# A fused attention and mixing kernel: the last two outputs of a step's second half are written to the tiles of the folds

## The reference, cut to what matters

```
# 1. attention, 8 heads of 64: a pooled softmax attention (tokens averaged in fours), repeated back,
#    plus a banded one (|i - j| < 4)                          -> x  [4, 576, 512]
# 2. mixing:
X = fft(fft(x, axis=1), axis=2);  u = x + real(X)
un = (u - mean(u)) / sqrt(var(u) + 1e-6)
y = u + relu(un @ w_ch1) @ w_ch2                  # w_ch1 512 x 2048, w_ch2 2048 x 512
# 3. gated convolution:
gate = sigmoid(5-tap causal convolution of y)
out = (gate * (y @ w_val)) @ w_out
```

## Time and profile before

| | us |
|---|---|
| median of 3 runs | 764.14 |
| lowest, highest of them | 763.96, 766.54 |
| the profiled execution's own time | 765.54 |
| its span, first to last instruction | 763.7 |

### The profile page before, as it was taken

One profiled execution on the slowest core, in us unless ns is written; L12 is line 12 of the kernel. 1 busy time (PEld: TensorE's weight loads), 2 busy tenths in 40 slices (PEclk: granted clock), 3 DMA queues, 4 the chain that ended last, 5 costly groups with the idle time before them and its releaser, 6 DMA issues.

```text
span 763.7 us, 14781 instructions
## 1 busy us (share of the span) xinstructions
PE 715.4 (94%) x5960; PEld 540.7 (71%) x5960; DVE 382.2 (50%) x925; ACT 193.6 (25%) x417; POOL 151.6 (20%) x131
## 2 busy tenths in 40 slices
PE   2579959999999998999999999999999999999998
PEld 1455646877767876877767877877767877777776
DVE  4457585554555852543555873543555851123452
ACT  1536531322212122222212132222212121111201
POOL 8001677991101211000201311000101300000000
PEclk9999858999999999999999999999999999999999
DMA  9994228022001036022000127022000000000001
GB/s 264 283 254 123 85 88 199 19 66 64 11 1 58 21 102 160 2 59 64 18 2 32 39 78 193 2 59 66 16 1 1 9 29 27 1 2 1 1 23 40
DMA packets 42246, 48.96 MB, mean 64 GB/s; under 512 B 4803, under 2 KB 35846, under 8 KB 41094
## 3 DMA queue, kind: packets, MB, share of 16 engines
q1 hardware_dynamic: 32608, 31.06, 16.0%
q10 hardware_dynamic: 9574, 16.99, 7.3%
HBM read 43.32 MB, written 4.72 MB: 63 GB/s over the span
## 4 chain that ended last, share of the span: by engine, by line
PE 85%; DVE 4%; DMA 3%; POOL 3%; issue 2%; ACT 2%; ACTq 1%; SPq 0%; POOLq 0%
PE Y L580 24%; PE P L563 24%; PE Y L685 4%; PE P L696 4%; PE P L685 4%; PE A L592 3%; PE Y L696 3%; PE A L646 2%; PE A L550 2%; DMA out<-ot 2%; PE A L543 2%; PE A L533 2%; PE A L635 1%; PE A L486 1%; PE P L543 1%
## 5 line engine op out<-in xcount | busy, mean ns | idle before, releaser
L563 PE MATMUL P<-unT,w_wv 128*128 128x288 f16 x1536 | 212.0, 289 | 3.9 <-DVE hT L1144 3.1
L580 PE MATMUL Y<-hT,w 128*128 128x288 f16 x1536 | 215.2, 287 | 0.0
L563 PEld LDWEIGHTS P<-unT,w_wv 128*128 128x128 f16 x1536 | 149.6, 99 | 49.1 <-issue 6.4
L1144 DVE SCALAR_TENSOR_TENSOR hT<-P,hT 128x288 f16<-128x288 f32 x128 | 58.4, 457 | 248.9 <-ACT hT L820 248.5
L580 PEld LDWEIGHTS Y<-hT,w 128*128 128x128 f16 x1536 | 146.3, 98 | 42.1 <-issue 5.3
L820 ACT ACTIVATE hT<-P 128x288 f16<-128x288 f32 x128 | 52.4, 411 | 212.3 <-PE P L563 210.7
L1180 DVE SCALAR_TENSOR_TENSOR gate<-xT,cw,gate 128x288 f32<-128x288 f32 x128 | 66.4, 519 | 4.5
L791 ACT ACTIVATE prob_or_un<-prob_or_un 73x288 f32<-73x288 f32 (+1 forms) x52 | 23.3, 448 | 88.5 <-DVE prob_or_un L1017 84.8
L1315 POOL MEMSET x<- 1x512 f32 x4 | 2.1, 517 | 209.0 <-ACT x L809 209.0
L696 PE MATMUL Y<-shared,wo 128*128 128x288 f32 x128 | 32.1, 409 | 0.5 <-DVE shared L1190 0.5
L696 PE MATMUL P<-shared,wo 128*128 128x288 f32 x128 | 31.8, 407 | 0.5 <-DVE shared L1190 0.5
(11 more groups left out here) (167 smaller groups left out, 839.3 us busy)
## 6 DMA issues: line engine op xcount, KB each, us to landing
kl<-qk_win SPq DMA_DIRECT2D x38, 140.0 KB, 6.5
ql<-qk_win SPq DMA_DIRECT2D x19, 256.0 KB, 4.4
vl<-v_win SPq DMA_DIRECT2D x72, 65.0 KB
pair_or_folded<-qk_pool SPq DMA_DIRECT2D x8, 580.0 KB, 5.8
pair_or_spectrum<-qk_pool SPq DMA_DIRECT2D x8, 580.0 KB, 6.3
out<-ot ACTq DMA_DIRECT2D x32, 144.0 KB, 1.8
w_wv<-w_ch ACTq DMA_DIRECT2D x4, 1024.0 KB, 11.7
w<-w_ch ACTq DMA_DIRECT2D x4, 1024.0 KB, 11.0
```

The lines of the kernel that those rows point to most:

```text
L563: last = mm(P[s % 2][:, 0:HN], w1s(k, f, wt), unT[:, ut, k, ha * HN:(ha + 1) * HN], start=k == 0 and wt + ut == 0, stop=k == KD - 1 and wt ...
L580: last = mm(Y[d][:, 0:HN], w2s(f, d, wt), hT[s % 3][:, ht, :], start=f == 0 and wt + ht == 0, stop=f == KF - 1 and wt == 1)
L1144: nc.vector.scalar_tensor_tensor(out=hT[s % 3][:, 1, :], in0=P[s % 2][:, 0:HN], scalar=0.0, in1=hT[s % 3][:, 0, :], op0=ALU.max, op1=ALU.s ...
```

## The change

`ot` gets two more entries, the first 288 columns of fa and of fb, and two more store semaphores. In the first half of a step blocks 0 to 3 use ot[0], ot[1], ot[0], ot[1] as before. In the second half they use ot[0], ot[1], fa and fb. The writes to fa and fb there have no wait of their own on ACT; the waits for their stores stand ahead of the first fold of the next image but one, on POOL for fa and on DVE for fb (only for images 2 and 3). The counts waited for in st_out[0] and st_out[1] become three uses an image, and SP's last wait covers four semaphores.

```diff
-        ot = [sb(f"ot{i}", [128, HN]) for i in range(2)]
+        ot = [sb(f"ot{i}", [128, HN]) for i in range(2)] + [fa[:, 0:HN], fb[:, 0:HN]]
-        st_out = [sem("st_out0"), sem("st_out1")]
+        st_out = [sem(f"st_out{i}") for i in range(4)]
-            sp.wait_ge(st_out[0], (B * 4 + 1) * 16)
-            sp.wait_ge(st_out[1], (B * 4 + 1) * 16)
+            sp.wait_ge(st_out[0], (B * 3 + 1) * 16)
+            sp.wait_ge(st_out[1], (B * 3 + 1) * 16)
+            sp.wait_ge(st_out[2], B * 16)
+            sp.wait_ge(st_out[3], B * 16)
@@ outputs(b, ha)
                     act.wait_ge(out_ps, n + 1)
-                    act.wait_ge(st_out[d % 2], 16 * (4 * b + 2 * ha + d // 2 + 1))
-                    nc.scalar.mul(ot[d % 2][:], (P[d % 2] if ha == 0 else Y[d])[:, 0:HN], 0.5).then_inc(out_sb, 1)
+                    i = d if ha == 1 else d % 2
+                    if i < 2:
+                        act.wait_ge(st_out[i], 16 * (3 * b + (2 if ha == 1 else d // 2) + 1))
+                    nc.scalar.mul(ot[i][:], (P[d % 2] if ha == 0 else Y[d])[:, 0:HN], 0.5).then_inc(out_sb, 1)
                     act.wait_ge(out_sb, n + 1)
-                    act.dma_start(out[b, d * 128:(d + 1) * 128, ha * HN:(ha + 1) * HN], ot[d % 2][:]).then_inc(st_out[d % 2], 16)
+                    act.dma_start(out[b, d * 128:(d + 1) * 128, ha * HN:(ha + 1) * HN], ot[i][:]).then_inc(st_out[i], 16)
@@ fold(b, i), on DVE
+                if i == 0 and later(b - 1):
+                    dve.wait_ge(st_out[3], 16 * (b - 1))
+                    dve.sem_inc(passed, 1)
@@ fold_even(b, i), on POOL
+                if i == 0 and later(b - 1):
+                    pool.wait_ge(st_out[2], 16 * (b - 1))
+                    pool.sem_inc(passed, 1)
```

## The result

| | before | changed | ratio, 95% interval |
|---|---|---|---|
| measured for the result | 767.25 us, median of 14 (763.96 to 770.74) | 762.89 us, median of 14 (760.59 to 765.77) | 0.9941, 0.9920 to 0.9961 |
| second time, other runs | 766.63, 35 runs | 763.86, 12 runs | 0.9954, 0.9932 to 0.9977 |
| third time | 765.61, 17 runs | 762.96, 12 runs | 0.9952, 0.9927 to 0.9976 |

The changed kernel is faster by 4.4 us in the first measurement, 2.8 and 2.7 in the later two, and by 3.9 us, 0.5%, on the mean of the three ratios. The forecast was 4.4 us off, but off 764.14, the median of three runs; over 14 runs the kernel before takes 767.25. So the absolute time, 762.89, lies outside the range that I gave (758.6 to 761.5).

The account below looks back on a forecast made before the run. PE was taken as the bound. Stalls of 2.46 and 0.95 us plus 1.68 of slow clock make 5.09; 4.4, the middle of 3.69 and 5.09, off the 764.14 median gives 759.7 us (-0.58%), range 758.6 to 761.5.

Parts of the forecast that it names:

- Cause, place and size of the stalls: Ends of step(1, 0) and step(2, 1): loads delay stores, ACT's relu comes late, PE stops 2.46 and 0.95 us.
- the stretch that I forecast as 170.3 us: Start of project(1) in one middle step to the next: both take 170.3 us after the change, against 174.40 and 171.22.
- The clock's 1.68 us: PE's matmuls after the stop at the end of step(1, 0) run at a lowered clock; 1.68 us goes with the stall.
- Costs put at nothing: Added POOL and DVE waits (0 to 0.64 us), ACT's issues beside four stores (0 to 0.1 each end): taken as 0.
- rival (c): ACT at both ends: a third or fourth store's issue waits for an earlier store; 761.1 us, chance 0.06.
- (d): Rival: stores moved earlier share DMA engines with the next image's loads, which reach pool_qk late; slower, chance 0.02.
- How the sum stands to the runs: Whole kernel: 5.09 or 3.69 us off the 764.14 median, depending where the profiled execution lost 1.40; middle 4.4, giving 759.7.
- rival (a): Stalls at the two step ends are smaller in most executions, 0.95 us each; gain 1.9, time 762.2 us, chance 0.13.

Follow-up runs that it names:

- loads_later: Kernel before with two buffers, SP issuing the next image's loads from load_pair(b, 2) on only after all outputs of the step are issued: 761.86 us, 0.9936.
- before_b: The kernel before, unchanged, profiled and measured again: 766.34 us, ratio 0.9993.
- waits_only: Kernel before with two buffers, plus only the added POOL and DVE waits ahead of the folds of images 2 and 3: 766.24 us, 0.9991.
- the relu kernels: Changed kernel with slot 0's relu repeated in three steps: 3 more 762.28 us; 7 more 772.22 and 770.66; 12 more 781.50; 7 more with loads held back 777.17.
- relu7_quiet: Changed kernel with seven more relus of slot 0 in three steps and SP's loads held until the next step's first mlp_down: 777.17 us, one run.
- relu_plus7_b: Changed kernel with seven more relus of slot 0 in three steps, an unchanged second execution: 770.66 us, one run.
- after_loads_later: Changed kernel plus SP's loads issued only after all outputs of the step are issued: 762.45 us, 0.9951 to the kernel before.
- third_only: Kernel before with one buffer more: only the second half's third block goes to fa, the fourth keeps ot[1]: 765.67 us, 0.9987.
- after_b: The changed kernel, unchanged, profiled and measured again: 763.86 us, 0.9954 to the kernel before.

## Why the prediction was right and where it was wrong

**Cause, place and size of the stalls: right.** They sit at the two ends that I named. Loads make the stores late (loads_later), ACT's order carries that to PE, and the loss is 5.09 us in the profile that I read, 5.87 in before_b and 5.04 in waits_only. The changed kernel has none of it, and the stretch that I forecast as 170.3 us is 170.26. This shows the stalls of the profiled executions. It doesn't show that they are as large on the average of all executions (see what stays open).

**The clock's 1.68 us: right that it goes with the stop.** The rows of one stop couldn't show it; the relu kernels do. But it doesn't come with every stop (last section).

**Costs put at nothing: right for PE.** The added waits cost POOL 0.19 us each, DVE and PE nothing that the rows show. Four stores in flight didn't hold ACT's issues, which are 0.34 to 0.35 us; rival (c) didn't occur. The loads weren't missed by pool_qk, whose only wait for a load is one of 1.3 us in the opening (1.4 before), so neither did (d). Of what the prediction takes from the Trainium skill, "DMA: Bandwidth & Descriptors", sections "Issuing engines are not separate DMA queues" and "Queues, rings and completion order", one part agrees with the rows: more buffers make no store land sooner, 5.7 to 7.0 us after and 5.9 before. The other part, that stores put earlier hold up the loads behind them, doesn't show: the windows of keys landed in 7.8 us after and 8.2 before, at the median of the same stretch. In loads_later, with fewer transfers side by side, the stores did land sooner.

**Wrong: "How the sum stands to the runs".** This is the step that failed. I took 4.4 us off 764.14 and gave 758.6 to 761.5. The 4.4 was met, 4.36 in the same measurement, and that is luck: it was the middle between two answers to a question that didn't exist, the stretches gave 5.1 in this profile, and the later measurements have 2.8 and 2.7. The base was not met. Three runs from 763.96 to 766.54 stood for a kernel whose 14 runs go to 770.74 with a median 3.1 us higher. My range held the doubt on the gain and none on the base. The question was where the profiled execution, 765.54 us, had lost its 1.40 us. Beside 767.25 it had lost nothing and was 1.7 us quick. The whole sum off that base, 767.25 - 5.09, is 762.2, 0.7 from what was measured. The profiles also show where executions differ most: not in the stalls. The opening varies from 279.3 to 284.1 us over fourteen profiles (relu7_quiet has 284.12), almost 5 us, while everything behind it repeats within 0.05 us in the changed kernel and 0.8 in the one before.

Where in the opening? The start of the first mlp_up, at the end of step(0, None), lies at 113.75 (relu_plus7_b) to 118.66 us (relu7_quiet), and from there to project(1) it is 165.3 to 166.7 us. So it is made mostly before 119 us, while weights and first windows are loaded. In thirteen of the fourteen profiles PE's scores of a window wait there for a load of keys, 2.5 to 6.3 us in all, with two buffers and with four; only the first profile of before, the one that I had read, has no such wait. Here waits_only and the changed kernel's first profile:

```profile
PE Y L479 <- DMA kl<-qk_win: 3.8, 1, 3.8
```

```profile
PE Y L481 <- DMA kl<-qk_win: 6.3, 2, 3.2
```

The size of this wait doesn't order the openings (3.3 us in the shortest, relu_plus7_b, and 2.5 in before_b, whose opening is 2.7 us longer), so it is not shown to be what makes the difference.

**What stays open.** Behind the opening the change is worth 5.3 us in the profiles, in the measured medians 2.7 to 4.4. The 38 runs of the changed kernel have a mean of 763.1 us, the 89 of the kernel before beside them 767.0: 3.9 us, with an interval of about 3.2 to 4.6, so the missing 1.4 us are more than noise. The three profiles of the changed kernel have openings of 283.3 to 283.7, the three with two buffers 280.6 to 282.0, which would make up for it. That the three are no chance can be estimated: an execution takes 1.8 us more than its span, and 763.1 - 1.8 - 478.06 leaves a mean opening of 283.2 us over all 38 runs. For the kernel before, 767.0 - 1.8 - 483.3 leaves 281.9, if the stalls are as in its profiles.

So there are two answers, and no run parts them. Either this kernel's opening is 1.3 us longer, or the stalls cost 3.9 us on the average and 5.3 in the three profiles, a mild form of rival (a); in all three the clock fell behind the first stop, and the relu kernels show that the same stop can leave it up. For the first answer there are also 12 runs of after_loads_later against 12 of loads_later, neither with a stall: by the same estimate openings of 282.9 and 281.6, within noise of each other. Against it, the five relu kernels hold the whole change and the same instructions in the opening, and have 279.38, 280.71, 279.29, 280.30 and 284.12, one execution each. The start of the first mlp_up, 116.0 us on the mean of the nine profiles that hold the whole change and 116.0 in the four without it (before, before_b, waits_only, loads_later), doesn't tell them apart either. Whether the change, or the place of its code in this one build, lengthens the opening is not shown.

## What to carry to other kernels

A wait in the list is worth what it keeps from the bounding engine, and what is late next bounds that: remove the wait that comes second in the same chain too, or little moves. Where a trace has the same work twice, once disturbed and once not, take the difference of the whole stretches; it gave the gain of these stretches in this profile to 0.1 us. It is one execution's gain: the mean of all runs moved by 3.9 us, not 5.1. A forecast of an absolute time must carry the spread of its base, and three runs don't show it: compare how long each part takes in several profiles, and forecast the ratio from the parts that repeat.

## What the runs showed of the hardware that I had not expected

**The clock behind a stop.** The granted clock was 1.00 while PE ran the 24 matmuls ahead of each stop. Behind eight stops of 0.79 to 2.25 us (start of the 12 matmuls, less the start of the 24, less 2.94) the clock never fell. Behind the twelve of 2.46 to 2.79 us it fell ten times, to windows of 0.50 to 0.85; two stops of 2.79 us, one with loads and one without, left it at 1.00. Behind the three of 4.98 us it fell each time. Within one execution the same stop gave both outcomes. So a stop a little shorter may save 1.7 us more than its own shortening. third_only, 2.25 us for 2.46, may be such a case, but with one execution that isn't shown; behind which stop the clock falls, these runs can't tell.

**DVE held by POOL.** loads_later's first stretch is 170.93 us and not 170.26. In it four instructions of the convolution took 4.34 us on DVE, from 444.19, while POOL's addition of the values (2.35 us) ran from 445.87. Three of the four took 0.52 us each, and the last, which began at 445.9 too, 2.68:

```profile
444.19 4.34 DVE L1183 SCALAR_TENSOR_TENSOR gate<-xT,cw,gate 128x288 f32<-128x288 f32 x4
445.87 2.35 POOL L1368 TENSOR_TENSOR prob_or_un<-prob_or_un 72x1024 f32<-72x1024 f32 x1 [11.36 <-DMA prob_or_un<-v_pool]
```

In after_b POOL began after DVE had ended, and the four took 2.18, 0.52 each:

```profile
446.18 2.18 DVE L1187 SCALAR_TENSOR_TENSOR gate<-xT,cw,gate 128x288 f32<-128x288 f32 x4
448.56 2.36 POOL L1375 TENSOR_TENSOR prob_or_un<-prob_or_un 72x1024 f32<-72x1024 f32 x1 [12.07 <-DMA prob_or_un<-v_pool]
```

The 2.16 us more on DVE are about the length of POOL's instruction. The gate then comes late, ACT's copies of the next transposes stand behind it, and PE is idle for 1.03 us between two groups of transposes where after_b has 0.36: the 0.67 us. The first profile of the changed kernel has the same, 4.33 us for four from 275.40 with POOL from 277.07, in its opening. The Trainium skill, "SBUF — State Buffer", section "SBUF: two separate sides", says that DVE and GpSimd share a pair of ports as an exclusive lock: for a DVE instruction with two inputs in SBUF and a GpSimd one that reads SBUF, as here, the first to start holds the pair for its whole instruction and the other "fully blocks". The rows agree with it; no run here tried it by itself.
